# Row-packed inverse products with zero-filled unused partitions, in a spectral mixer followed by a two-layer feed-forward network

## The reference

```python
X = np.fft.rfft(x, axis=1)
Xr, Xi = X.real, X.imag
Yr = Xr @ w_r - Xi @ w_i + b_r
Yi = Xr @ w_i + Xi @ w_r + b_i
Yr = np.sign(Yr) * np.maximum(np.abs(Yr) - 0.01, 0.0)     # and Yi alike
y = np.fft.irfft(Yr + 1j * Yi, n=3008, axis=1)
h = y.reshape(12032, 256) @ w_in
g = np.maximum(h, 0.0) + alpha * np.minimum(h, 0.0)
return g @ w_out
```

## Time and profile before

| | |
|---|---|
| median of 3 runs | 1421.91 us (1421.27 to 1425.54) |
| profiled execution, time | 1423.1 us |
| its span, first to last instruction | 1421.3 us |
| PE, busy | 1391.1 us (98%) |
| PE weight loads, busy | 1168.1 us (82%) |
| DVE, busy | 949.9 us (67%) |
| ACT, busy | 744.2 us (52%) |
| POOL, busy | 306.7 us (22%) |

### The profile page before, as it was taken

One profiled execution on the slowest core, in us unless ns is written; L12 is line 12 of the kernel. 1 busy time (PEld: TensorE's weight loads), 2 busy tenths in 40 slices (PEclk: granted clock), 3 DMA queues, 4 the chain that ended last, 5 costly groups with the idle time before them and its releaser, 6 DMA issues. The chain is left out here.

```text
span 1421.3 us, 21507 instructions
## 1 busy us (share of the span) xinstructions
PE 1391.1 (98%) x7012; PEld 1168.1 (82%) x7012; DVE 949.9 (67%) x1824; ACT 744.2 (52%) x1646; POOL 306.7 (22%) x351
## 2 busy tenths in 40 slices
PE   7999999999999999999999999999999999999997
PEld 4887888888888888888888888888888888888886
DVE  5785767878765557877775656787776555555554
ACT  3774555656644545656654455565654444444433
POOL 0442532222201422222210241222220010001000
PEclk9997999999999999999999999999999999999999
DMA  6643532221210432213211243222121011101101
GB/s 214 195 150 107 152 93 57 69 64 53 63 36 18 128 109 61 67 47 79 57 34 39 60 115 75 57 68 62 52 56 34 19 32 26 19 14 32 21 15 15
DMA packets 163114, 94.68 MB, mean 67 GB/s; under 512 B 110500, under 2 KB 140628, under 8 KB 163004
## 3 DMA queue, kind: packets, MB, share of 16 engines
q1 hardware_dynamic: 158250, 88.91, 23.8%
q10 hardware_dynamic: 4754, 4.41, 1.0%
HBM read 55.74 MB, written 37.49 MB: 66 GB/s over the span
## 5 line engine op out<-in xcount | busy, mean ns | idle before, releaser
L1008 DVE SCALAR_TENSOR_TENSOR g_raw<-negpart,keep,h_ps 128x502 f32<-128x502 f32 (+1 forms) x384 | 282.5, 736 | 374.4 <-ACT negpart L785 368.6
L785 ACT ACTIVATE negpart<-h_ps 128x502 f32<-128x502 f32 (+1 forms) x384 | 225.1, 586 | 471.3 <-PE h_ps L461 470.9
L461 PE MATMUL out_ps<-g_hi,wout_hi 128*128 128x502 f32 (+1 forms) x768 | 312.7, 407 | 6.8 <-DVE g_lo L911 4.9
L461 PE MATMUL h_ps<-y_hi,win_hi 128*128 128x502 f32 (+1 forms) x768 | 300.7, 392 | 0.2 <-DVE y_lo L911 0.2
L461 PE MATMUL h_ps<-y_lo,win_hi 128*128 128x502 f32 (+1 forms) x768 | 300.6, 391 | 0.0
L461 PE MATMUL h_ps<-y_hi,win_lo 128*128 128x502 f32 (+1 forms) x768 | 299.8, 390 | 0.0
L461 PE MATMUL out_ps<-g_hi,wout_lo 128*128 128x502 f32 (+1 forms) x768 | 299.4, 390 | 0.0
L461 PE MATMUL out_ps<-g_lo,wout_hi 128*128 128x502 f32 (+1 forms) x768 | 298.3, 388 | 0.0
L911 DVE TENSOR_TENSOR g_lo<-g_raw,g_hi 128x502 fp32r<-128x502 f32 (+1 forms) x384 | 271.0, 706 | 0.1
L794 ACT ACTIVATE g_hi<-g_raw 128x502 fp32r<-128x502 f32 (+1 forms) x384 | 236.0, 615 | 0.3 <-DVE g_raw L1008 0.3
L461 PEld LDWEIGHTS out_ps<-g_hi,wout_hi 128*128 128x128 f32 x768 | 144.7, 188 | 40.4 <-DVE g_lo L911 10.9
(11 more groups left out here) (117 smaller groups left out, 1984.1 us busy)
## 6 DMA issues: line engine op xcount, KB each, us to landing
pair_raw<-fwd_scratch SPq DMA_DIRECT2D x96, 128.0 KB, 2.1
back_raw<-inv_scratch SPq DMA_DIRECT2D x61, 192.0 KB, 2.5
table<-in_twiddles_dram SPq DMA_DIRECT2D x28, 384.0 KB, 3.4
x_raw<-in_x_dram SPq DMA_DIRECT2D x64, 160.0 KB
inv_scratch<-inv_sb SPq DMA_DIRECT2D x36, 256.0 KB, 2.2
fwd_scratch<-staging SPq DMA_DIRECT2D x44, 192.0 KB, 2.0
out_dram<-turned SPq DMA_DIRECT2D x124, 40.0 KB, 2.0
inv_scratch<-inv_sb SPq DMA_DIRECT2D x24, 128.0 KB, 2.7
```

The lines of the kernel that those rows point to most:

```text
L461: mm = pe.matmul(ps, lhs, rhs, start=(first and n == 0), stop=(last and n == len(terms) - 1), **kw)
L785: act.activation(negpart[:, q % 2, 0:size], h_ps[:, q % 2, 0:size], ACT.Relu, scale=-1.0).then_inc(negpart_done, 1)
L1008: dve.scalar_tensor_tensor(g_raw[:, q % 2, 0:size], negpart[:, q % 2, 0:size], keep[:, m:m + 1], h_ps[:, q % 2, 0:size], ALU.mult, ALU.add ...
```

## The change

- `inverse1`, for the 122 units inside the tiles: three products instead of four. `back_hi` has 128 rows: rows 0 to 95 are the hi parts, rows 96 to 127 the lo parts of rows 0 to 31. The second operand has the matching rows of `idft` again. The lo parts of rows 32 to 95 of both b stand in one 128-row weight tile (`back_lo`), taken once against `idft_rest`, 2 x 94 columns with zeros where the other b's rows are.
- The lo parts are made by two engines: DVE has a new operation `rest_first(v)`, 32 x 512, in step 4j + 3 behind `g_lo` (and behind `x_hi` where there is one); POOL's `rest_back` takes 128 x 256 instead of 96 x 512. ACT has one more copy, 128 x 256, behind `back_hi` in step 4j + 2.
- `inverse1` waits for `rest_first` of its pair (`back_part_done`); so does the next `load_back`.
- `load_back` issues four transfers instead of one: the 96 rows, rows 0 to 31 again, and rows 32 to 95 for each b.
- `dft` has 128 x 128 elements, `x_hi` and `x_lo` 128 rows, the unused ones zero: `forward1` is 128 x 128 weights against 512 columns. The six units in the head have 128 rows too, with zeros below row 96, and their six products each. At the start DVE clears rows of `x_hi` and `x_lo`, POOL rows of `back_hi`, `back_lo` and `idft_parts`. ACT issues one load of `dft` instead of two, and makes one more copy (`idft_rest`).
- `y_part` now lies in `bias`, whose value is no longer used by then.

```diff
             def load_back(v):
                 sp.wait_ge(back_lo_done, v)
+                if v > HEAD_V:
+                    sp.wait_ge(back_part_done, v - HEAD_V)
...
                              inv_dram[g, :, b:b + 2, :]).then_inc(back_loaded, 16)
+                sp.dma_start(back_raw[ROWS:P, :].rearrange("r (b d) -> r b d", b=2),
+                             inv_dram[g, 0:P - ROWS, b:b + 2, :]).then_inc(back_loaded, 16)
+                for k in range(2):
+                    sp.dma_start(inv_sb[64 * k:64 * k + 64, 2, :],
+                                 inv_dram[g, P - ROWS:ROWS, b + k, :]).then_inc(back_loaded, 16)
...
             def inverse1(u):
                 pe.wait_ge(back_lo_done, v + 1)
+                if v >= HEAD_V:
+                    pe.wait_ge(back_part_done, v - HEAD_V + 1)
...
+                if u >= I_HEAD:
+                    for b in range(2):
+                        d = slice(b * DIM + h * P, b * DIM + (h + 1) * P)
+                        pe.matmul(i_bank(u)[:, b * 2 * NA:(b + 1) * 2 * NA], back_hi[:, v % 2, d], parts,
+                                  start=b == 0, stop=False, skip_group_check=True)
+                    pe.matmul(i_views(u)[0], back_lo[:, v % 2, h * P:(h + 1) * P], idft_rest[:, :, :],
+                              start=False, stop=True, skip_group_check=True).then_inc(back_mm, 1)
+                    return
...
             def split_back(v):
-                act.activation(back_hi[:, v % 2, :], back_place(v), ACT.Copy).then_inc(back_hi_done, 1)
+                act.activation(back_hi[:, v % 2, :], back_raw[:, :], ACT.Copy)
+                act.activation(back_lo[:, v % 2, DIM:2 * DIM], inv_sb[:, 2, :], ACT.Copy).then_inc(back_hi_done, 1)
...
+            def rest_first(v):
+                dve.wait_ge(back_hi_done, v + 1)
+                rest(back_hi[ROWS:P, v % 2, :], back_raw[ROWS:P, :], back_hi[ROWS:P, v % 2, :]).then_inc(back_part_done, 1)
...
             def rest_back(v):                                  # POOL
                 pool.wait_ge(back_hi_done, v + 1)
-                rest(back_lo[:, v % 2, :], back_place(v), back_hi[:, v % 2, :]).then_inc(back_lo_done, 1)
+                rest(back_lo[:, v % 2, 0:DIM], inv_sb[:, 2, :], back_lo[:, v % 2, DIM:2 * DIM]).then_inc(back_lo_done, 1)
```

More of the change, by code:

```diff
@@ L110, in mixer_kernel @@
         room = sb("room", [P, 7 * P])
-        dft_raw, idft_raw = room[0:NA, 0:ROWS], room[0:ROWS, ROWS:ROWS + NA]
+        dft_raw, idft_raw = room[:, 0:P], room[:, P:P + 3 * NA]
         spec = room[:, 0:2 * P].rearrange("p (h w c) -> p h w c", h=DH, w=2)
@@ L125, in mixer_kernel @@
         x_raw = sb("x_raw", [NA, X_RING, 2 * DIM])
-        x_hi, x_lo = (sb(f"x_{h}", [NA, 2, 2 * DIM], F32R) for h in ("hi", "lo"))
+        x_hi, x_lo = (sb(f"x_{h}", [P, 2, 2 * DIM], F32R) for h in ("hi", "lo"))
         staging = sb("staging", [ROWS, OUT_RING, 2 * DIM])
@@ L140, in mixer_kernel @@
         inv_sb = sb("inv_sb", [P, 3, DIM])
-        back_raw = sb("back_raw", [ROWS, 2 * DIM])
-        back_hi, back_lo = (sb(f"back_{h}", [ROWS, 2, 2 * DIM], F32R) for h in ("hi", "lo"))
-        y_part = sb("y_part", [P, 2 * NA])
+        back_raw = sb("back_raw", [P, 2 * DIM])
+        back_hi, back_lo = (sb(f"back_{h}", [P, 2, 2 * DIM], F32R) for h in ("hi", "lo"))
+        y_part = bias[:, 0:2 * NA]
         y_hi, y_lo = (sb(f"y_{h}", [P, DH, HALF], F32R) for h in ("hi", "lo"))
@@ L231, in back_place @@
         def back_place(v):
-            return negpart[0:ROWS, v - 1, :] if v in (1, 2) else back_raw[:, :]
+            return negpart[0:ROWS, v - 1, :] if v in (1, 2) else back_raw[0:ROWS, :]
         def back_arrived(eng, v):
@@ L561, in inverse1 @@
                     both = i_bank(u)[:, b * 2 * NA:(b + 1) * 2 * NA]
[L562 to L569, removed]
+                    hi, lo = back_hi[:, v % 2, d], back_lo[:, v % 2, d]
+                    mm = product(both[:, 0:NA], [(hi, parts[:, 0:NA]), (hi, parts[:, NA:2 * NA]), (lo, parts[:, 0:NA])])
                 mm.then_inc(back_mm, 1)
@@ L770, in split_back @@
                     act.wait_ge(back_mm, 2 * v - 2)
-                act.activation(back_hi[:, v % 2, :], back_place(v), ACT.Copy).then_inc(back_hi_done, 1)
+                if v < HEAD_V:
+                    act.activation(back_hi[0:ROWS, v % 2, :], back_place(v), ACT.Copy).then_inc(back_hi_done, 1)
+                    return
+                act.activation(back_hi[:, v % 2, :], back_raw[:, :], ACT.Copy)
+                act.activation(back_lo[:, v % 2, DIM:2 * DIM], inv_sb[:, 2, :], ACT.Copy).then_inc(back_hi_done, 1)
             def split_y(u):
@@ L801, in split_ffw @@
                                ACT.Copy).then_inc(wout_hi_done, 1)
-            for first, end in ((0, 80), (80, NA)):
-                act.dma_start(dft_raw[first:end, :], dft[first:end, :]).then_inc(dft_loaded, 16)
+            act.dma_start(dft_raw, dft).then_inc(dft_loaded, 16)
             act.dma_start(idft_raw, idft).then_inc(idft_loaded, 16)
@@ L815, in _ @@
                     act.wait_ge(idft_loaded, 16)
-                    act.activation(idft_parts[:, 0, :], idft_raw, ACT.Copy).then_inc(hi_const, 1)
+                    act.activation(idft_parts[:, 0, :], idft_raw[:, 0:NA], ACT.Copy)
+                    act.activation(idft_rest[:, :, :].rearrange("p b a -> p (b a)"), idft_raw[:, NA:3 * NA],
+                                   ACT.Copy).then_inc(hi_const, 1)
                 if s == 10:
@@ L1058, in turn @@
                 op.then_inc(turned_done, 1)
+            for t in (x_hi, x_lo):
+                dve.memset(t[64:P, :, :].bitcast(F32), 0.0).then_inc(x_zero, 1)
             dve.wait_ge(hi_const, 1)
@@ L1112, in _ @@
                         split_x(s_unit(f, m + 2), False)
+                    v = i_bpair(f, m - 3)
+                    if v is not None:
+                        rest_first(v)
                     p = p_couple(f, m, 3)
@@ L1196, in rest_wout @@
                      wout_hi[:, w, :, :].rearrange("p m e -> p (m e)")).then_inc(wout_lo_done, 1)
+            pool.memset(idft_parts[ROWS:P, 1, :].bitcast(F32), 0.0).then_inc(lo_zero, 1)
+            for t in (back_hi, back_lo):
+                pool.memset(t[ROWS:P, :, :].bitcast(F32), 0.0).then_inc(back_zero, 1)
+            pool.wait_ge(back_zero, 2)
             rest_tw(0)
```

41 lines of the change are left out of this document (27 added, 14 removed).

## The result

| | before | after |
|---|---|---|
| median | 1421.59 us (4 runs, 1418.38 to 1425.54) | **1430.93 us** (4 runs, 1428.30 to 1432.62) |
| ratio, with 95% interval | | 1.0066 (1.0049 to 1.0083) |
| profiled execution: time, span | 1423.1, 1421.3 | 1428.3, 1426.5 |

The change made the kernel 0.66% slower, 9.3 us by the medians. The forecast was 1425 and the range 1412 to 1434 holds the time, but the sign that the forecast gave the most weight, no measurable difference, is not what came.

A forecast was written before the change was run, and what follows sets the result against it. PE, busy 98% of the span, was taken as the bound. From 1421.9 us, -13.7 for saved products and +5.3, +9.3, +1.0, +1.5 for stalls gave +3.4, so 1425; range 1412 to 1434.

The forecast's parts named there:

- no measurable difference: Whole kernel: the measured time cannot be told from no change, within about 0.3% (4.3 us); chance 0.45.
- The product taken out: PE, tiles: 122 units lose one weight load of 0.1125 us each, 13.7 us less.
- The plain pairs: 25 pairs in plain steps: PE waits 0.21 us each for `rest_first` behind `g_lo`, 5.3 us more.
- The late pairs: 12 pairs where DVE already lags: nine cost PE 9.3 us, the first tile's three 1.0 together.
- the three kinds: Late pairs recurring in each of three batches: PE's load moves 1.0, 1.4 and 0.7 us later.
- The covered pairs: 24 pairs with other PE work around the unit keep the whole gain; three with full DVE lists cost 1.5 us together.
- tile 4 and its likes: Three covered pairs where DVE's list is full: 0 to 0.69 us each at PE's next wait, 0.5 taken.
- ACT, POOL, SP and traffic: ACT's copy, POOL's shorter operation, SP's four transfers and memory traffic: nothing on the path, no time added.
- The sum: Whole kernel: -13.7 + 5.3 + 9.3 + 1.0 + 1.5 = +3.4 us on 1421.9, giving 1425; bounds 1416.7 to 1431.7.
- Rival 1: Tiles: with `rest_first` done in 0.45 us or PE 0.2 later, the plain pairs cost nothing; 1414; chance 0.20.
- Rival 3: Loaded stretches: DVE and POOL get in each other's way in 36 pairs, 10 us slower, 1435; chance 0.15.
- Rival 2: Head: `forward1`'s 128 x 128 weights may let the clock rise earlier; 1422, down to 1419; chance 0.20.

The follow-up runs named there:

- e4: The changed kernel without DVE's `rest_first` and the waits for it; tiles 11.0 us shorter than before the change, 23.6 shorter than after.
- e5: The changed kernel with `rest_first` working in place on rows 0 to 31 instead of 96 to 127; median 3.0 us shorter than the changed kernel's.
- e8: e3 with a semaphore behind ACT's first copy, so that `rest_first` can start 0.4 us earlier; the time is e3's.
- e10: e7 with DVE making both lo parts and POOL none; the time is e7's.
- e3: The changed kernel with `rest_first` at the end of DVE's step 4j + 2 instead of in step 4j + 3; 1414.85 us.
- e7: e3 with ten more idle-filling products in two places of the head where PE idled; 0.9938 of the kernel before.
- e12: The kernel before with only the columns of `dft` padded with zeros, 94 x 128 weights, rows still 94; 1.0008 of the kernel before.

## Why the prediction was right and where it was wrong

- **The product taken out, -13.7.** Right. A unit step that meets no wait is 0.109 us shorter (76 of them here, 112 in e4), against 0.1125 forecast.
- **The plain pairs, +5.3.** Right mechanism and right count, size off. All 25 pairs waited, 0.32 us each instead of 0.21: 7.9 us. The step that failed is "less the 0.08 by which neighbours on DVE overlap": that is so between operations that start on the same rows, not for one that starts on row 96. e5 puts the 0.21 back (0.19).
- **The late pairs, +9.3 with 1.0 for the first tile.** Right. With the product given back (0.11 each) the three kinds cost 0.96, 1.48 and 0.71; forecast 1.0, 1.4, 0.7.
- **The covered pairs, +1.5.** The place "tile 4 and its likes" was right and 0.93 for each lies above the bound of 0.69: `room` (L961) starts 1.67 us behind the start of its step's `hidden`, where it was 0.83 before, and PE waits at the end of the chain behind it (0.92 at 370.28). The three steps at 243, 585 and 927 (1.9 us) were overlooked: there is no unit in them, only the list of DVE one step on.
- **ACT, POOL, SP and traffic at nothing.** Right within 2.4 us (e4).
- **The sum.** Tiles +3.4 forecast, +12.6 measured: the 9.2 between them are 2.6 from the plain pairs, 0.9 from the second units at 247 and their likes, 1.3 from tile 4's steps, 1.9 from those at 243, 1.1 spread over 252 steps, 1.0 from six loaded units, and 0.4 of small rests. So the plain stall, mis-sized by 0.11, is the largest single miss and under a third of the whole; most of the rest is DVE's list in the loaded steps, where the forecast had a wait in too few places.
- **Rival 1** fell: no plain pair was without its wait. **Rival 3** fell as a mechanism: in the changed kernel `rest_first`'s mean is 0.69 and `g_lo`'s 0.71 (0.71 before), and e8 and e10 gained nothing. Its time, 1435, was the nearest all the same, by luck. **Rival 2** came true on top of the sum, about 3 us by the medians; a chance was given to it alone, and I should have added it to the cases.
- So the time fell between two errors: the head's gain of some 3 us, left out of the forecast, and 9 us too little of stalls in the tiles. That the range holds the time is in part luck. Without the head, the sum's own upper bound, 1431.7, would have been passed (1421.9 + 12.6 = 1434.5).

## What to carry over

An operation that is moved to another engine is placed by the list, not by the load: 0.69 us on an engine busy 67% of the time cost 23.6 us behind one instruction and, by e3, at most 7 one step earlier, where that engine was idle. Before costing a new wait, look for the idle gap ahead of the chain that the waiting engine follows; if there is one, put the work there, and the same change that lost 0.66% gains 0.6% (e7: 0.9938, the best of the complete kernels, level with e10). And where a forecast rests on how closely two operations follow one another, check that they start on the same partitions.

## What the runs showed of the hardware

- A DVE operation that starts on row 96 behind one on row 0 starts 0.03 us behind its end; one that starts on row 0 too starts 0.08 ahead of it.
- POOL takes 0.77 us for 128 x 256 and 1.29 us for 32 x 512; DVE takes 0.41 to 0.42 and 0.69. Both go by the columns, not by the rows.
- DVE's 32 x 512 and POOL's 128 x 256 side by side take 0.92 and 1.00 us.
- Products of 94 rows, 0.43 us apart and back to back for 20 us, left PE at 1.2 GHz; products of 128 rows, 34 of them zero, had it at 2.4 GHz by 12 us. The granted clock's row reads 1.00 in both (this for the kernel before): where a trace starts at the low clock, the distance of the products tells, not that row.

```profile
10.00:20.00 10.00, 9.92 (x23) 4.72 (x22) 7.50 (x15) 4.11 (x9) 0.00 (x0) 1.00 0.90 274
```

- Behind two waits of 0.7 us the clock can fall. In e3 two waits, at 637.1 and 638.5, are followed by products 0.42 apart:

```profile
638.49 0.50 PE L475 MATMUL out_ps<-g_hi,wout_hi 128*128 128x502 f32 x1 [0.73 <-DVE g_lo L937]
...
639.10 0.62 PE L475 MATMUL out_ps<-g_hi,wout_lo 128*128 128x502 f32 x1
639.52 0.62 PE L475 MATMUL out_ps<-g_hi,wout_hi 128*128 128x502 f32 x1
```

That step is 1.37 us longer than in before, where the same two waits (0.7 for `pair_lo`, 0.7 for `g_lo`) stand and the clock holds. The nine stretches of half clock in the tiles of seven traces all stand right behind these two waits, which come three times in every kernel here, 42 times in the 14 traces; e12, whose tiles are those of before, has one. Why it falls in nine of the 42 isn't known. Part of the 7 us by which the runs of one kernel differ may come from there; that isn't shown.
